# State products in four quarters, logits summed beside the turn of x, maxima joined on GpSimd, more of w1a loaded in the attention

## The chip, the cores and the metric

The kernel runs on one core of a Trainium2 chip. Its time is the device time of one execution in microseconds; the median of three runs stands for it. TensorE is called PE, VectorE DVE, ScalarE ACT, GpSimd POOL; SyncE (SP) issues nearly all loads.

## What is computed

Three layers follow one another, all in float32 at the outside.

```python
# 1. retention: 4 sequences, 8 heads, 768 tokens, 64 values a head
state = gamma[h] * state + outer(k[t], v[t])        # per head, 64 x 64
y[t] = q[t] @ state / sqrt(64)
x = y as (3072 tokens, 512)
# 2. soft mixture: 8 experts of 4 slots
logits = x @ phi                                    # 3072 x 32
d = softmax(logits, over the tokens); c = softmax(logits, over the slots)
slot_in = d.T @ x                                   # 32 x 512
slot_out[e] = relu(slot_in[e] @ w1[e]) @ w2[e]      # w1a, w2a in the kernel
x = c @ slot_out
# 3. top-2 mixture of 8 experts with noisy gates
out = sum of the two chosen experts' relu(x @ w1[e]) @ w2[e], weighted   # w1b, w2b
```

## The kernel before

**Tiling.** Tokens go in NT = 24 chunks of P = 128, six (NC) a sequence. Layer 1 works a chunk at a time: scores of keys against queries within the chunk, masked; the decayed v by the masked scores (`probs`), plus the state by the queries; then the state's update. Heads lie in pairs: partitions 0 to 63 hold the even head of pair n, 64 to 127 the odd one, so a state product contracts 64 rows into 64 columns.

**Order on TensorE.** It is written out by hand in `sequence_products` (L735). Step t does, in this order: `scores` of chunk t+1 (L643), `logit_parts_of` chunk t-1 (L657: phi by x, one part for each 128 values, in four column groups of 32), `turn_x` of t-1 (L675, four transposes, behind a wait for the state), at a few steps `turn_max` (L704) and `spread_max` (L710), `outputs` of t (L684 the state products, L690 v by probs), `logit_rows` of t-1 (L664, which adds the four parts by a stack of unit matrices), `update` of t (L697; not for a sequence's last chunk). In three steps `slot_sums` and `den_sums` (L719, L731) follow: sums over the tokens of exp(logits) by x, for one group of chunks. There are five groups (0 to 3, 4 to 7, 8 to 13, 14 to 19, 20 to 23), each with the running maximum of its columns; older sums are faded to the new maximum.

**Other engines in a step.** DVE: scales and decays the output into `x_t` (L1189), brings the state forward (L1198, L1201), masks the scores of t+2 (L1182). The column maximum of a group is four things: a reduce and a copy on DVE (L1222, L1224), a transpose on PE, a reduce, a join and a diagonal on DVE (L1230 to L1233), a product on PE that spreads it, then the shift (L1241). ACT copies the parts (L1009), the turned x (L1015) and the logits (L1017) out of the PSUM banks, and takes the exponentials. POOL decays v of t+2 once chunk t's v is used up (`decay_chunk`, L531), in a loop of the engine, and is free of other work until the attention ends. Its first partition all-reduce stands in `w2b_all_sum` (L564).

**Loads.** All go through one SP queue in the order of the program: for each chunk g the queries and keys half (`load_qk`) and the turned keys and v half (`load_kv`), 512 KB each, as soon as their buffers are free (four and two deep: the second waits for scores and the decay of v of chunk g-2), and behind them halves of w1a's units, 1 MB each, evenly spread: 14 over the chunks 3 to 23. A unit is 2 MB, 16 KB in each of 128 partitions; `w_region` holds eight, `s_region` two. The eighth unit of w1a has its home in unit 3, where the attention keeps its input chunks, so its second half is loaded when those two buffers are free and the first half after the last scores. Then come w2a's units (their homes are freed by the w1a products, `ring_used`), w1b's and w2b's.

**Behind the attention.** The w1a products (L808), the w2a products (L830), the softmax over the slots and the gates, the choice of two experts and sorting of tokens, mostly on DVE, the w1b weights folded with the slots (L866), and a loop over RT = 55 tiles (L940, L957) in which POOL fetches records and writes and adds rows by indirect transfers (L588, L594, L600).

## Time and profile before

| | us |
|---|---|
| timed, median of three runs (564.08 to 568.5) | 565.28 |
| span of the profiled execution | 563.3 |
| PE busy | 515.7 (92%) |
| DVE busy | 277.4 (49%) |
| POOL busy | 257.3 (46%) |
| ACT busy | 187.4 (33%) |
| moved by the DMA engines | 107.91 MB, mean 192 GB/s |

The profile is one execution. Its views show busy time in stretches, instructions in order of time with the idle time ahead of them and what ended it, and the chain of work that ended last. A product in float32 is two instructions in the profile. The DMA share is the mean busy share of 16 DMA engines. The attention runs from about 5 us to 134 us, the w1a and w2a products to 185 us, gates and sorting to 241 us, the tile loop to the end.

### The profile page before, as it was taken

The page shows a single profiled execution, that of the slowest core. Times are in us where ns is not written, and L with a number is a line of the kernel's source. Part 1 is how long each engine was busy: PE and PEld are TensorE (multiplying, and loading weights), DVE is VectorE, ACT ScalarE, POOL GpSimd, SP SyncE. Part 2 cuts the span into 40 slices and gives each one's busy share as a digit, 9 for nine tenths or more (in the row PEclk, how much of TensorE's full clock was granted, in tenths as well). Part 3 has the DMA queues.
Part 4 walks back from the last instruction along what each step waited for, and adds up shares of the span by engine and source line. Part 5 has one row for each costly group of instructions (what it writes and reads, how often), then busy time and mean ns, then how long its engine had stood idle before and what let it go on. Part 6 is the DMA issues. An engine that isn't in the chain of part 4 may idle for free.

```text
span 563.3 us, 13506 instructions
## 1 busy us (share of the span) xinstructions
PE 515.7 (92%) x4845; PEld 305.0 (54%) x4846; DVE 277.4 (49%) x449; ACT 187.4 (33%) x345; POOL 257.3 (46%) x216
## 2 busy tenths in 40 slices
PE   4999999998895767789999999999999999999992
PEld 4787878775465534345545454545454545454541
DVE  1665756573710388863363637373737242424240
ACT  0122222222000354763636464545452222222220
POOL 1212221220100003735587778777778757566632
PEclk9999999999799578979999999999999999999998
DMA  7899999877899999915435552222232342424310
GB/s 261 308 324 392 313 353 340 334 287 266 347 430 424 427 400 412 311 50 200 156 94 177 191 189 44 41 40 54 42 54 43 49 56 42 57 38 54 45 18 2
DMA packets 32358, 107.91 MB, mean 192 GB/s; under 512 B 11567, under 2 KB 12831, under 8 KB 27840
## 3 DMA queue, kind: packets, MB, share of 16 engines
q1 hardware_dynamic: 18144, 92.89, 43.5%
q0 software_dynamic: 14176, 14.49, 14.3%
q8 instruction: 26, 0.43, 0.3%
q14 instruction: 12, 0.10, 0.1%
HBM read 93.87 MB, written 29.43 MB: 219 GB/s over the span
## 4 chain that ended last, share of the span: by engine, by line
PE 82%; DVE 7%; DMA 4%; issue 3%; ACT 1%; POOL 1%; SPq 0%; DVEq 0%; POOLq 0%
PE ps L957 49%; PE ps L940 4%; PE ps L690 4%; PE ps L643 4%; PE ps L684 3%; PE ps L808 3%; PE ps L830 3%; PE ps L675 3%; PE ps L697 2%; DMA w_region<-chunks 2%; DMA w_region<-moe_w 2%; PE ps L664 1%; PE ps L657 1%; PE ps L719 1%; ACT r_region L1067 1%
## 5 line engine op out<-in xcount | busy, mean ns | idle before, releaser
L957 PE MATMUL ps<-w_region,s_region 128*128 (+1 forms) x1320 | 296.1, 381 | 1.1 <-ACT s_region L1136 1.1
L957 PEld LDWEIGHTS ps<-w_region,s_region 128*128 128x128 f16 x1320 | 127.4, 98 | 145.7 <-issue 4.2
L1559 DVE SCALAR_TENSOR_TENSOR s_region<-ps,s_region 128x1024 f16<-128x1024 f32 x55 | 67.3, 1224 | 148.4 <-ACT s_region L1136 148.3
L1136 ACT ACTIVATE s_region<-ps 128x1024 f16<-128x1024 f32 x55 | 56.3, 1023 | 183.2 <-PE ps L940 178.8
L594 POOL DMA_INDIRECT out<-s_region,rec_region x41 | 56.1, 1367 | 53.2 <-DVE s_region L1588 50.0
L600 POOL DMA_INDIRECT out<-s_region,rec_region x42 | 67.8, 1614 | 16.4 <-issue 12.0
L588 POOL DMA_INDIRECT rec_region<-records,idx x55 | 60.0, 1090 | 24.9 <-issue 16.3
L531 POOL TENSOR_TENSOR s_region<-w_region,s_region 128x512 f32<-128x512 f32 x22 | 22.9, 1042 | 90.5 <-PE ps L697 71.7
L940 PEld LDWEIGHTS ps<-s_region,sw_region 128*128 (+1 forms) x440 | 29.4, 98 | 15.3 <-issue 2.7
L1588 DVE TENSOR_SCALAR s_region<-ps,rec_region,y_scale 128x512 f32<-128x512 f32 x42 | 33.8, 804 | 6.9 <-PE ps L957 5.4
L940 PE MATMUL ps<-s_region,sw_region 128*128 128x128 f16 x440 | 34.1, 221 | 2.0 <-ACT sw_region L1089 2.0
L1189 DVE TENSOR_TENSOR sw_region<-ps,s_region 128x512 f32<-128x512 f32 x24 | 16.6, 692 | 35.0 <-PE ps L690 35.0
L1360 DVE SCALAR_TENSOR_TENSOR w_region<-w_region,w2b_scale 128x2048 f16<-128x2048 f32 x14 | 32.6, 2342 | 0.0
L564 POOL PARTITION_ALL_REDUCE w2b_sum<-w2b_sum x8 | 3.2, 402 | 56.6 <-ACT w_region L1067 55.9
L1049 ACT ACTIVATE w_region<-w_region,w2b_scale 128x2048 f16<-128x2048 f32 x14 | 27.8, 2001 | 0.7 <-DVE w2b_scale L1354 0.7
L594 POOL DMA_INDIRECT out<-r_region,rec_region x13 | 19.5, 1504 | 16.4 <-DVE r_region L1588 15.6
L1009 ACT ACTIVATE s_region<-ps 128x128 f32<-128x128 f32 x24 | 6.7, 277 | 52.8 <-PE ps L657 52.8
L1067 ACT ACTIVATE r_region<-w_region 128x2048 f16<-128x2048 f32 x12 | 22.9, 1912 | 0.5 <-DMA w_region<-moe_w 0.4
L600 POOL DMA_INDIRECT out<-r_region,rec_region x13 | 20.7, 1592 | 4.8 <-issue 3.7
L643 PE MATMUL ps<-w_region 64*128 64x128 f32 x192 | 15.8, 310 | 5.1 <-DMA w_region<-chunks 5.0
L1182 DVE TENSOR_TENSOR sw_region<-ps,s_region 128x512 f32<-128x512 f32 x24 | 15.4, 680 | 9.2 <-PE ps L643 9.2
L1182 DVE TENSOR_TENSOR s_region<-ps,s_region 128x512 f32<-128x512 f32 x24 | 15.4, 681 | 6.5 <-PE ps L643 6.5
(241 smaller groups left out, 576.4 us busy)
## 6 DMA issues: line engine op xcount, KB each, us to landing
w_region<-moe_w SPq DMA_DIRECT2D x11, 2048.0 KB, 10.0
w_region<-chunks SPq DMA_DIRECT2D x34, 512.0 KB, 6.5
w_region<-moe_w SPq DMA_DIRECT2D x16, 1024.0 KB, 9.2
w_region<-moe_w SPq DMA_DIRECT2D x24, 512.0 KB, 17.1
s_region<-moe_w SPq DMA_DIRECT2D x4, 2048.0 KB, 16.8
sw_region<-chunks SPq DMA_DIRECT2D x12, 512.0 KB, 6.2
s_region<-moe_w SPq DMA_DIRECT2D x2, 1024.0 KB, 8.0
s_region<-moe_w SPq DMA_DIRECT2D x1, 1536.0 KB, 6.5
```

The lines of the kernel that those rows point to most:

```text
L588: nc.gpsimd.indirect_dma_start(rec_i[:, i * RW:(i + 1) * RW], None, records[:, :], bass.IndirectOffsetOnAxis(ap=idx[:, i:i + 1], axis=0), ...
L594: nc.gpsimd.indirect_dma_start(out[:, :], bass.IndirectOffsetOnAxis(ap=rec_i[:, i * RW + SL + 1:i * RW + SL + 2], axis=0), y_sb[i % DEPTH] ...
L600: nc.gpsimd.indirect_dma_start(out[:, :], bass.IndirectOffsetOnAxis(ap=rec_i[:, i * RW + SL + 2:i * RW + SL + 3], axis=0), y_sb[i % DEPTH] ...
L643: last = nc.tensor.matmul(bank[SC[c % 2][i]][:, n * P:(n + 1) * P], kt_in[g % KV_DEPTH][rows, n, :], qt_in[g % QK_DEPTH][rows, n, :], star ...
L940: last = nc.tensor.matmul(bank[2 + 2 * r + f // 4][:, f % 4 * P:(f % 4 + 1) * P], sw_parts[:, bass.ds(e, 1), f * P:(f + 1) * P].rearrange( ...
L957: last = nc.tensor.matmul(bank[6 + r], h[:, r, f, :], w2b_parts[:, bass.ds(o, 1), part, f, :].rearrange("p e m -> p (e m)"), start=(first ...
L1067: nc.scalar.activation(unused, w2b_in[e][:, part * UNIT // W2B_SUMS:(part + 1) * UNIT // W2B_SUMS], ACT.Abs, accum_out=w2b_sum[:, 0, e, pa ...
L1136: nc.scalar.activation(h_hi[:, r, :, :].rearrange("p c t -> p (c t)").rearrange("p (a n) -> p a n", a=2), ps[:, 2 + 2 * r:4 + 2 * r, :], A ...
L1182: last = nc.vector.tensor_tensor(probs[c % 2][:, i, :, :], bank[SC[c % 2][i]][:, :].rearrange("p (n t) -> p n t", n=NP), causal[:, :].unsq ...
L1360: last = nc.vector.scalar_tensor_tensor(out=w2b_parts[:, e, 1, chunks, :], in0=w2b_in[e].rearrange("p (c m) -> p c m", c=FC)[:, chunks, :] ...
L1559: nc.vector.scalar_tensor_tensor(out=h_lo[:, r, :, :].rearrange("p c t -> p (c t)").rearrange("p (a n) -> p a n", a=2), in0=ps[:, 2 + 2 * ...
L1588: nc.vector.tensor_scalar(y_sb[r], bank[6 + u % 2], rec[:, bass.ds(i * RW + SL, 1)], y_scale[:, bass.ds(o, 1)], ALU.mult, ALU.mult).then_i ...
```

## The change

- **Quarters.** The output of the attention lies in two PSUM banks, Y and Y+1, 256 columns each, instead of one. The state product of head (row half i, pair n = 2m + half) goes to column half `half` of bank Y + i, so that four products in a row use four different 64x64 quarters of the array. The values of x come out in another order; the constants, phi and w1a's rows are laid out to match on the host.
- **Logits.** The parts lie beside the outputs in bank Y+1, the row sums beside the state in bank ST. The row sum of chunk t-2 follows the turn of x of chunk t-1 (before: that of t-1 followed the outputs of t), from one of two buffers. The wait for the state moves from ahead of the turn to behind it. New waits: the outputs wait for the copy of the parts, the update for the copy of the logits, ACT for the older row sum.
- **Maxima.** DVE's reduce is followed by one partition all-reduce on POOL (in the order of `decay_chunk`, behind chunks 6, 10, 16 and 22, whose loop is now unrolled, and once after the attention), DVE's maximum with the older one and the shift. The fade comes from the difference of two maxima, picked by three small DVE operations behind the shift. PE's transpose and spread go.
- **Loads.** A new region `late_w1a` of 12 KB a partition takes three quarters of w1a's eighth unit in two pieces (1 MB and 512 KB) spread with the others, 16 pieces over the chunks 3 to 23; the last quarter is loaded to unit 3 when its buffers are free. Behind the last scores, where w1a's half was loaded, three quarters of w2a's eighth unit are loaded to unit 3; only its last quarter waits for the w1a products.
- **Rings.** The space that POOL's transfers are described in (`dynamic_dma_scratch_size`) is set to 4 KB a partition, which makes room for the region.

The core of the diff; the rest follows from it (names of semaphores, buffers, and the waits ahead of the w1a and w2a products).

```diff
...
+        LATE = 3 * UNIT // 4
...
+        late_w1a = sb("late_w1a", [P, LATE], F32)
...
-        Y, ST, T_X, LG = range(4, 8)
+        Y, T_X, ST = 4, 6, 7
+        y_of = [bank[Y + i][:, 0:2 * P] for i in range(2)]
+        y_all = ps[:, Y:Y + 2, 0:2 * P]
+        parts_at = bank[Y + 1][:, 2 * P:3 * P]
+        den_at = bank[Y + 1][:, 400:402]
+        state_at = bank[ST][:, 0:NP * D]
+        rows_at = bank[ST][:, NP * D:NP * D + SL]
...
-                more = (g - 2) * 2 * (E - 1) // (NT - 3)
+                more = (g - 2) * 2 * E // (NT - 3)
                 for half in range(ahead, more):
-                    w1a_half(half // 2, half % 2, w1a_early)
+                    if half < 2 * (E - 1):
+                        w1a_half(half // 2, half % 2)
+                    elif half == 2 * (E - 1):
+                        late_w1a_words(0, HALF)
+                    else:
+                        late_w1a_words(HALF, LATE)
                 ahead = more
...
-            w1a_half(E - 1, 1, w1a_last_full)
+            sp.dma_start(w1a_home[E - 1][:, LATE:UNIT], w1a[E - 1, :, LATE:UNIT]).then_inc(w1a_last_full, 16)
             sp.wait_ge(scores_ready, NT)
             sp.wait_ge(v_decayed, NT)
-            w1a_half(E - 1, 0, w1a_last_full)
+            load_w2a_words(E - 1, 0, LATE)
...
-            for c in range(2, NC):
-                decay_chunk(0, c)
-            with pool.Fori(1, B) as b:
-                for c in range(NC):
-                    decay_chunk(b, c)
+            def join_col_max(g):
+                pool.wait_ge(col_max_ready, g + 1)
+                nc.gpsimd.partition_all_reduce(col_max[:, 1 if g > 0 else 2, :], col_max[:, 0, :], P, MAX).then_inc(col_max_joined, 1)
+
+            for t in range(2, NT):
+                decay_chunk(t // NC, t % NC)
+                for g in group_ending(t - 2):
+                    join_col_max(g)
...
             pool.wait_ge(x_turned, NT)
             nc.gpsimd.memset(in_blocks, 0.0).then_inc(blocks_zeroed, 1)
+            join_col_max(NG - 1)
...
-            def logit_rows(b, c):
-
-                pe.wait_ge(parts_kept, b * NC + c + 1)
-                nc.tensor.matmul(bank[LG][:, P:P + SL], logit_parts, stack, start=True, stop=True).then_inc(logits_done, 1)
...
+            def logit_rows(t):
+
+                pe.wait_ge(parts_kept, t + 1)
+                if t > 0:
+                    pe.wait_ge(logits_kept, t)
+                nc.tensor.matmul(rows_at, logit_parts[t % 2], stack, start=True, stop=True).then_inc(logits_done, 1)
...
             def outputs(b, c):
 
+                t = b * NC + c
+                if t > 0:
+
+                    pe.wait_ge(parts_kept, t)
                 if c > 0:
-                    for n in range(NP):
-                        for i in range(2):
-                            part = slice(i * D, (i + 1) * D)
-                            nc.tensor.matmul(bank[Y][part, n * P:(n + 1) * P], state[part, n, :],
-                                             qt_in[(b * NC + c) % QK_DEPTH][part, n, :],
-                                             start=(n == 0), stop=False, skip_group_check=True)
-                pe.wait_ge(v_decayed, b * NC + c + 1)
-                pe.wait_ge(probs_ready, b * NC + c + 1)
+                    for m in range(2):
+                        for half in range(2):
+                            for i in range(2):
+                                rows, n = slice(i * D, (i + 1) * D), 2 * m + half
+                                nc.tensor.matmul(y_of[i][half * D:(half + 1) * D, m * P:(m + 1) * P], state[rows, n, :],
+                                                 qt_in[t % QK_DEPTH][rows, n, :],
+                                                 start=(m == 0), stop=False, skip_group_check=True)
+                pe.wait_ge(v_decayed, t + 1)
+                pe.wait_ge(probs_ready, t + 1)
+                for m in range(2):
+                    for i in range(2):
+                        for half in range(2):
+                            n = 2 * m + half
+                            h = 2 * n + i
+                            last = nc.tensor.matmul(y_of[i][half * D:(half + 1) * D, m * P:(m + 1) * P],
+                                                    v_dec[c % 2][:, h * D:(h + 1) * D], probs[c % 2][:, i, n, :],
+                                                    start=(c == 0 and m == 0), stop=(m == 1), skip_group_check=True)
+                last.then_inc(y_ready, 1)
+
+            def update(b, c):
+                t = b * NC + c
+                if t > 1:
+
+                    pe.wait_ge(logits_kept, t - 1)
                 for h in range(H):
-                    last = nc.tensor.matmul(bank[Y][h % 2 * D:(h % 2 + 1) * D, h // 2 * P:(h // 2 + 1) * P],
-                                            v_dec[c % 2][:, h * D:(h + 1) * D], probs[c % 2][:, h % 2, h // 2, :],
-                                            start=(c == 0 and h < 2), stop=(h >= H - 2), skip_group_check=True)
-                last.then_inc(y_ready, 1)
-
-            def update(b, c):
-                for h in range(H):
-                    last = nc.tensor.matmul(bank[ST][h % 2 * D:(h % 2 + 1) * D, h // 2 * D:(h // 2 + 1) * D],
-                                            k_in[(b * NC + c) % QK_DEPTH][:, h * D:(h + 1) * D], v_dec[c % 2][:, h * D:(h + 1) * D],
+                    last = nc.tensor.matmul(state_at[h % 2 * D:(h % 2 + 1) * D, h // 2 * D:(h // 2 + 1) * D],
+                                            k_in[t % QK_DEPTH][:, h * D:(h + 1) * D], v_dec[c % 2][:, h * D:(h + 1) * D],
                                             start=(h < 2), stop=(h >= H - 2), skip_group_check=True)
                 last.then_inc(update_done, 1)
...
-                    if c > 0 or b > 0:
-                        logit_parts_of(before_b, before_c)
-                        if c > 0:
-
-                            pe.wait_ge(state_ready, b * (NC - 1) + c)
-                        turn_x(before_b, before_c)
-                    t = b * NC + c
-                    for g in group_ending(t - 1):
-                        turn_max(g)
-                    for g in group_ending(t - 2):
-                        spread_max(g)
+                    logit_parts_of(t - 1)
+                    turn_x(t - 1)
+                    if c > 0:
+
+                        pe.wait_ge(state_ready, b * (NC - 1) + c)
+                    if t > 1:
+                        logit_rows(t - 2)
                     outputs(b, c)
-                    if c > 0 or b > 0:
-                        logit_rows(before_b, before_c)
                     if c < NC - 1:
-                        for g in group_ending(t - 1) + (group_ending(t - 2) if c == 0 else []):
-
-                            pe.wait_ge(max_diag_ready, g + 1)
-                        for g in group_ending(t - 2) + (group_ending(t - 3) if c == 0 else []):
-
-                            pe.wait_ge(cols_shifted, g + 1)
                         update(b, c)
                     for g in group_ending(t - 3):
                         if g < NG - 2:
                             slot_sums(g, range(GROUPS[g][1] - GROUPS[g][0]), bank[T_X], t)
...
-            logit_parts_of(B - 1, NC - 1)
-            turn_x(B - 1, NC - 1)
-            logit_rows(B - 1, NC - 1)
-
-
-            slot_sums(NG - 2, range(REP), bank[0], GROUPS[NG - 2][1])
-            turn_max(NG - 1)
-            slot_sums(NG - 2, range(REP, GROUPS[NG - 2][1] - GROUPS[NG - 2][0]), bank[0], GROUPS[NG - 2][1])
+            logit_parts_of(NT - 1)
+            logit_rows(NT - 2)
+            turn_x(NT - 1)
+            logit_rows(NT - 1)
+
+
+            slot_sums(NG - 2, range(GROUPS[NG - 2][1] - GROUPS[NG - 2][0]), bank[0], GROUPS[NG - 2][1])
             den_sums(NG - 2, NT)
...
+            def keep_logits(t):
+                act.wait_ge(logits_done, t + 1)
+                nc.scalar.activation(logits[:, t, :], rows_at, ACT.Copy).then_inc(logits_kept, 1)
+
+            def keep_chunk(t):
+                act.wait_ge(parts_done, t + 1)
+                if t > 1:
+
+                    act.wait_ge(logits_done, t - 1)
+                nc.scalar.activation(logit_parts[t % 2], parts_at, ACT.Copy).then_inc(parts_kept, 1)
                 for n in range(NG - 2):
-                    if GROUPS[n][0] == g - len(x_ring):
+                    if GROUPS[n][0] == t - len(x_ring):
 
                         act.wait_ge(slot_in_done, n + 1)
-                act.wait_ge(x_turned, g + 1)
-                nc.scalar.activation(x_home(g), bank[T_X][:, :], ACT.Copy).then_inc(x_kept, 1)
-                act.wait_ge(logits_done, g + 1)
-                nc.scalar.activation(logits[:, g, :], bank[LG][:, P:P + SL], ACT.Copy).then_inc(logits_kept, 1)
+                if t == NT - 1:
+                    keep_logits(t - 1)
...
+                if 0 < t < NT - 1:
+                    keep_logits(t - 1)
...
+            def max_at(g):
+                return col_max[:, 2 + g % 2, :]
+
+            def shift_cols(g):
+                dve.wait_ge(col_max_joined, g + 1)
                 if g > 0:
+                    link(nc.vector.tensor_tensor(max_at(g), col_max[:, 1, :], max_at(g - 1), ALU.max))
                 if 0 < g < NG - 1:
 
                     dve.wait_ge(den_kept, g)
                 nc.vector.tensor_tensor(exp_of(g), logits[:, GROUPS[g][0]:GROUPS[g][1], :],
-                                        bank[ST][:, 3 * P:3 * P + SL].unsqueeze(1)
-                                        .to_broadcast([P, GROUPS[g][1] - GROUPS[g][0], SL]),
+                                        max_at(g).unsqueeze(1).to_broadcast([P, GROUPS[g][1] - GROUPS[g][0], SL]),
                                         ALU.subtract).then_inc(cols_shifted, 1)
+                if g > 0:
+                    dve.wait_ge(ident_full, 16)
+                    link(nc.vector.tensor_tensor(gap_stack, max_at(g - 1), max_at(g), ALU.subtract))
+                    link(nc.vector.tensor_tensor(gap_stack, gap_stack, stack, ALU.mult))
+                    nc.vector.tensor_reduce(gap[:, g:g + 1], gap_stack, AX_X, ALU.add).then_inc(gap_found, 1)
...
-                        join_max(g)
+                        find_max(g)
                     for g in group_ending(t - 2):
                         shift_cols(g)
                     keep_x_t(b, c)
-                    for g in group_ending(t):
-                        find_max(g)
...
-    y_decay = (power / np.sqrt(D)).reshape(H // 2, 2, 1, P).repeat(D, 2).reshape(H // 2, P, P).transpose(1, 0, 2)
+    y_decay = (power / np.sqrt(D)).reshape(H // 4, 2, 2, P).transpose(1, 2, 0, 3)[:, None].repeat(D, 1).reshape(P, H // 2, P)
...
-    nc = bacc.Bacc("TRN2", target_bir_lowering=False, num_devices=1)
+    nc = bacc.Bacc("TRN2", target_bir_lowering=False, num_devices=1, dynamic_dma_scratch_size=4096)
...
+    for name in ("moe_phi", "moe_w1"):
+        arrays[name] = by_quarter(arrays[name], inputs["q"].shape[1])
...
```

## Rows read from the trace of the kernel before

**Rows 1.** Windows: us, busy (instructions) by engine, PEclk, DMA share, GB/s.

```profile
20.00:120.00 100.00, 99.40 (x1495) 78.44 (x1491) 62.39 (x111) 22.08 (x66) 20.71 (x20) 1.00 0.95 348
20.00:30.00 10.00, 9.83 (x154) 7.81 (x152) 6.58 (x10) 2.14 (x6) 2.08 (x2) 1.00 1.00 387
150.00:182.50 32.50, 25.18 (x676) 19.19 (x669) 5.56 (x20) 0.87 (x2) 0.00 (x0) 1.00 1.01 426
```

**Rows 2.** The chain that ended last, tile loop: start us, us, what.

```profile
307.67 5.18 PE ps L957 x24
...
313.35 5.18 PE ps L957 x24
```

**Rows 3.** Timeline of step 3: start us, us, engine line op, shapes [idle before <-releaser].

```profile
26.57 1.16 PE L643 MATMUL ps<-w_region 64*128 64x128 f32 x16
...
27.15 0.97 DVE L1201 TENSOR_TENSOR s_region<-s_region 128x256 f32<-128x256 f32 x1
...
28.17 0.42 PEld L675 LDWEIGHTS ps<-ident_stack,sw_region 128*128 128x128 f32 x4 [0.35 <-DVE s_region L1201]
...
28.76 0.85 PEld L684 LDWEIGHTS ps<-sw_region,s_region 64*64 64x64 f32 x16 [0.17 <-issue]
...
29.78 1.09 PE L690 MATMUL ps<-s_region 128*64 128x128 f32 x16
...
30.81 0.41 PE L664 MATMUL ps<-ident_stack,s_region 128*128 128x32 f32 x2
...
31.14 0.69 PE L697 MATMUL ps<-s_region,sw_region 128*64 128x64 f32 x16
...
31.76 0.38 PE L643 MATMUL ps<-w_region 64*128 64x128 f32 x2
```

**Rows 4.** The chain that ended last, w2a products (L830).

```profile
161.78 5.45 PE ps L830 x192
...
170.06 3.70 PE ps L830 x128
...
182.47 2.36 PE ps L830 x36
```

**Rows 5.** The chain that ended last, end of the attention.

```profile
121.12 0.11 PE ps L704
...
124.23 1.09 PE ps L643 x16
...
126.36 0.33 PE ps L710 x2
...
133.42 0.70 DVE sw_region L1189
...
143.26 2.77 PE ps L808 x21
```

**Rows 6.** POOL's timeline, and the instructions of L543 and L564 (ns min/median/max).

```profile
10.15 0.28 POOL L543 TENSOR_SCALAR_AFFINE_SELECT before<-before 128x128 f32<-128x128 f32 x1 [8.71 <-issue]
...
37.11 1.04 POOL L531 TENSOR_TENSOR s_region<-w_region,s_region 128x512 f32<-128x512 f32 x1 [4.08 <-PE ps L697]
...
L543 POOLq MODIFY_POOL_CONFIG  x2: 11/11/11, 1.5 to 1.5; - x2
...
L564 POOL PARTITION_ALL_REDUCE w2b_sum<-w2b_sum x8: 312/323/872, 198.2 to 408.3; - x8
L564 POOLq MODIFY_POOL_CONFIG  x2: 11/14/16, 142.5 to 142.5; - x2
```

**Rows 7.** The page's DMA issues: count, size of one, median us to landing.

```profile
w_region<-chunks SPq DMA_DIRECT2D x34, 512.0 KB, 6.5
```

**Rows 8.** POOL's timeline in the tile loop.

```profile
302.46 1.59 POOL L600 DMA_INDIRECT out<-s_region,rec_region  x1 [1.79 <-DMA out<-s_region,rec_region]
304.35 1.05 POOL L588 DMA_INDIRECT rec_region<-records,idx  x1 [0.30 <-issue]
305.71 1.04 POOL L594 DMA_INDIRECT out<-s_region,rec_region  x1 [0.30 <-issue]
```

More of the change, by code:

```diff
@@ L98, in build_program @@
         ident_at = y_dec_at + NP * P
-        logit_parts = work_tile(3, P)
+        logit_parts = [work_tile(3, P) for _ in range(2)]
         x_ring = [w_region[:, 7 * UNIT + i * DM:7 * UNIT + (i + 1) * DM] for i in range(UNIT // DM)] + [work_tile(3, DM)]
@@ L436, in _, with w1a_half, late_w1a_words @@
             HALF = UNIT // 2
-            def w1a_half(e, half, full):
+            def w1a_half(e, half):
                 words = slice(half * HALF, (half + 1) * HALF)
-                sp.dma_start(w1a_home[e][:, words], w1a[e, :, words]).then_inc(full, 16)
+                sp.dma_start(w1a_home[e][:, words], w1a[e, :, words]).then_inc(w1a_early, 16)
+            def late_w1a_words(first, last):
+                sp.dma_start(late_w1a[:, first:last], w1a[E - 1, :, first:last]).then_inc(w1a_early, 16)
             ahead = 0
@@ L645, in scores, with logit_parts_of @@
                 last.then_inc(scores_ready, 1)
-            def logit_parts_of(b, c):
-                pe.wait_ge(x_t_ready, b * NC + c + 1)
-                if not (isinstance(b, int) and b * NC + c == 0):
-                    pe.wait_ge(logits_kept, b * NC + c)
-                for g in group_ending(b * NC + c - 3):
+            def logit_parts_of(t):
+                pe.wait_ge(x_t_ready, t + 1)
+                if t > 0:
+                    pe.wait_ge(parts_kept, t)
+                for g in group_ending(t - 3):
                     if g < NG - 2:
@@ L722, in slot_sums, with den_sums @@
                     last.then_inc(slot_in_done, 1)
-            def den_sums(g, kept):
-                pe.wait_ge(logits_kept, kept)
+            def den_sums(g, read):
+                pe.wait_ge(x_t_ready, read)
                 if g == NG - 1:
@@ L730, in den_sums @@
                 for c in range(end - first):
-                    last = nc.tensor.matmul(bank[LG][c % REP * SL:(c % REP + 1) * SL, 480:482], exp_of(g)[:, c, :],
+                    last = nc.tensor.matmul(den_at[c % REP * SL:(c % REP + 1) * SL, :], exp_of(g)[:, c, :],
                                             ones[:, 0:2], start=(c < REP), stop=(c >= end - first - REP))
@@ L825, in _ @@
                 for f in range(FC):
-                    if e == E - 1 and f == FC // 2:
+                    if e == E - 1 and (f + 1) * DM > LATE:
                         pe.wait_ge(w2a_last_full, 16)
```

101 lines of the change are left out of this document (42 added, 59 removed).

## The prediction

> **What bounds the kernel now.** I read the windows first, then the timeline of one step, then the chain. From 20 to 120 us TensorE is busy 99.40 of 100 us [rows 1]: the attention is a TensorE loop with no hole. The same row has the DMA engines at 0.95, moving 348 GB/s. So the first question is not what TensorE saves but what the loads allow. Behind the attention the order turns round: the DMA share is 1.01 at 426 GB/s from 150 to 182.5, with TensorE busy 25.18 of 32.50 us [rows 1]. The products with w2a wait for their weights there. In the last stretch, the loop over 55 tiles, TensorE takes one tile per 5.68 us (307.67 to 313.35) [rows 2], and the change does not touch it.
>
> **One step of the attention.** Starts in [rows 3]: scores and logit parts 1.61 us, turn of x 0.58, state products 1.02, v by probs 1.03, logit rows 0.33, update 0.62, together 5.19. Three prices are read off it. A change of the tile shape costs an idle 0.17 (ahead of L684). The turn waits 0.35 for the state on VectorE (L675), 0.18 more than such a switch. Sixteen 64x64 state products take 1.02 us, 64 ns each, two running side by side.
>
> **Part 1, state products in quarters.** The sixteen instructions stay; their order and banks make four neighbours use four different quarters (row half i, column half `half`, bank Y+i). The trace has no four 64x64 quarters at once. The nearest row is four column groups of 32: 128 products of 128 columns in 3.70 us, 28.9 ns each [rows 4]. Sixteen by 28.9 ns are 0.46 us; I take 0.49 with the last one's tail, a saving of 0.53. The other end is no overlap beyond today's two: saving 0. I take the upper one, because the nearest row has the same columns and type. VectorE reads 512 columns a chunk as before, now from two banks, at the same 0.69 us, and waits for nothing new.
>
> **Part 2, logits.** The row sum (L664) of the chunk before goes right behind the turn, which has its shape, so one 0.17 switch of the 0.33 disappears; I take 0.15. Its input was copied a step ago. New on TensorE's queue is the wait of the outputs for ScalarE's copy of the parts, which lies under the turn's 0.58; ScalarE is busy only 22.08 of 100 us [rows 1]. If that cover went, 0.1 to 0.3 a step. The wait for the state now stands behind the turn instead of ahead of it, so the 0.17 or so goes too: VectorE finished at 28.12, the turn ends at 28.76 [rows 3]. With steps 0.85 shorter it still fits, since parts and turn follow the scores.
>
> An ordinary step is then 5.19 - 0.53 - 0.15 - 0.17 = 4.34 us of TensorE. Up to the last scores at 124.23 [rows 5] there are 18 steps with state products (9.5 us), 20 row sums (3.0), about 15 waits for the state (2.6). Part 3 adds 1.4. Sum 16.5: **by TensorE alone the last scores would start at 107.7.**
>
> **Part 3, maxima on POOL.** Three spreads of 0.33 (the fourth is in the tail) and four turns of 0.11 leave TensorE's queue [rows 5]: 1.4 us. VectorE loses copies and the join and gains three small operations behind the shift, under 0.8 us in front of x in four steps, which its idle time takes (62.39 of 100 us busy [rows 1]). Added on POOL is a partition all-reduce, 0.3 to 0.9 us, and something that comes ahead of the first one. The trace has two events that reconfigure POOL: at 1.5, after which its next instruction starts at 10.15 behind 8.71 us of idle time, and at 142.5, ahead of the first all-reduce, where a 56 us wait hid it [rows 6]. In the changed kernel the second comes in the middle of the attention. Queued behind it are the decay of v for chunk 7 (which frees the load of chunk 9) and, by the join, VectorE's shift and its x of chunk 6. Worked out: decay 6 ends at 38.15 today [rows 6], about 35.6 once four steps have saved their part, plus 8.7 is 44.3, all-reduce, shift and x end at 45.8; TensorE would want that x at 43.6. A stall of 2.2 us, once. Loads already queued cover some; I count 1.6. The bounds are 0 (if the load takes under 6.5 us) and 2.2.
> The Trainium skill, GPSIMD Engine Reference, 2.1 Instruction dispatch, says that the first call of a freshly loaded kernel pays about 6 us (5.95 measured) of code load with no visible instruction. By it the stall would be nil and the sum 1.6 us better; the row here has 8.71, and the row decides.
>
> **Part 4, three quarters of w1a's eighth unit early.** Ahead of the last chunk the SP queue now carries 15 pieces of w1a instead of 13, 2.1 MB more. So from 20 us on, 34.8 + 2.1 = 36.9 MB must land before the last scores. What rate? The whole 100 us gave 348 GB/s at 0.95, or 366 at a full share. But the ten microseconds with the engines full (20 to 30) gave 387, and 150 to 182.5 gave 426 [rows 1]. A half-megabyte load takes 6.5 us from issue to landing [rows 7], far more than its bytes need, so a share counted busy with few loads queued need not mean a full pipe. With loads always queued I take 395, nearer to the 387, since the mix is the same; 366 and 426 are the ends. 36.9 MB / 395 GB/s = 93.4 us: landed at 113.4, with 1.0 for the hand-over 114.4, with POOL's 1.6 **116.0**. That is later than TensorE's 107.7, so the loads decide, and the gain at the last scores is 124.2 - 116.0 = 8.2 us rather than 16.5.
> The tail from there to the last x is 9.9 us now (124.23 to 134.12) [rows 5]; two state products (1.06), one spread (0.33) and two row switches (0.3) leave it: 1.7. **The attention ends 9.9 us earlier.**
>
> **Behind the attention.** 1.57 MB of w1a no longer need moving there: in their place and time w2a's eighth unit loads, whose three quarters the stretch at 1.01 is then spared. 1.57 MB / 426 GB/s = 3.7 us. The path of the last maxima loses a turn and a spread (0.11 and 0.33) and two small operations of VectorE, about 1.2 us in all, but it ends at TensorE's w1a products, and what ends last is the w2a load, so I count 0. Check that TensorE doesn't become the bound: its w1a products would start 11 us before 143.26 [rows 5], its w2a products 11 us before 161.78, and the latter (eight times 64 at 28.9 ns, 14.8 us, and 0.8 for turns between) could end at 166.4, 18 us before 184.8; the loads allow 13.6 [rows 4]. What follows (gates, choice, records, second weights, 54 more tiles) shifts whole.
>
> **Rings of 4 KB.** By its name the space holds what POOL's own transfers need. Per tile POOL has 1.59 + 1.05 + 1.04 us and three gaps of 0.30, 4.6 of 5.68 us [rows 2, 8]. Room: 1.1 us a tile. I count 0; the cover is that room.
>
> **Sum.** 9.9 + 3.7 = 13.6. The profiled execution's span is 563.3, 2.0 below the median of the runs, 565.28; 549.7 of span, 551.7 timed.
>
> **Rivals.**
> *The loads hold at 366 GB/s.* For it: it is the rate of the whole stretch. Against: 387 and 426 in full windows. 36.9/366 = 100.8, so landed at 121.8, last scores at 124.4 or, with no stall, 122.8; gain 0 to 1.4, tail 1.7, w2a 3.7: about 559.
> The Trainium skill, DMA: Bandwidth & Descriptors, Where 436 GB/s comes from, says that HBM to SBUF is held to about 358 GB/s a core by HBM. That would be this rival, slightly worse; the trace's 426 over 32 us speaks against it for a single running core.
> *TensorE is the bound.* With 426 GB/s the loads land at 106.6, under TensorE's 107.7; with the stall 109.9, a gain of 14.3, then 1.7 and 3.7: 545.6. For it: the 426 of [rows 1], reached where loads are always queued. Against: over half of the bytes are chunk loads, which wait for buffers.
> *The quarters don't overlap.* TensorE alone: 124.2 - 7.0 = 117.2, with the stall 118.8; gain 5.4, tail 0.6, w2a 3.7: 555.6. It would be the change not doing what it says.
> *The attention gets no shorter*, because w1a's larger share ahead of the chunks in one queue delays them step by step: only 3.7 and perhaps 1: 561.
> *Slower: the small rings stall POOL.* If an indirect transfer has to wait for an earlier one's landing, and it costs POOL over 1.1 us a tile, each further microsecond is 54 us: with 1.79 (L600 waited that long for a DMA once already [rows 8]) 0.7 x 54 = 38, some 590. It decides from 1.1 us a tile; taken with the gain, from 1.35. Nothing else shows how full the rings are. A half clock in the attention would be slower too, but TensorE keeps a granted clock of 1.00, the 2.4 GHz level, in the window with 25.18 of 32.50 busy [rows 1], and the changed attention would leave it over 90% busy.
>
> **How the numbers follow.** Forecast (547 to 555) 0.45; quarters don't overlap 0.07; loads at 366 0.17; TensorE bound 0.12; attention no shorter 0.07; rings 0.07; slower otherwise 0.05. Leaving out the rings, the other slow cases and the lower end of the TensorE case, the range is 545 to 561. A per cent, 5.65 us, is about what a measurement of this kernel can tell. Faster than 559.6: 0.45 + 0.07 + 0.12 + half of the 366 case, 0.72. Within: the other half and the 561 case, 0.16. Slower 0.12.
>
> **What would show it.** In the profile after: L684's group at about 30 ns per instruction; an ordinary step of TensorE near 4.4 us of work inside a step of 4.6, with idle ahead of the scores put down to the chunk loads; a share of 0.99 or more and 385 to 405 GB/s from 20 to 110; one hole of 1 to 3 us near 44, with POOL idle some 8 us ahead of its first all-reduce; the last scores near 116; the w2a products' end at 171 instead of 184.8; POOL's rows in the tile loop unchanged. It is wrong if the scores don't wait for loads (then TensorE case), if the rate at full share stays below 375, or if tiles take over 5.68 us.

## The result and the profile after

| | before | after |
|---|---|---|
| median of the runs (lowest to highest), us | 564.68 (561.9 to 568.5, 4 runs) | 593.63 (591.25 to 596.68, 4 runs) |
| ratio to before, 95% interval | 1 | 1.051 [1.046, 1.057] |
| span of the profiled execution, us | 563.3 | 595.0 |
| mean granted clock of TensorE | 0.96 | 0.935 |

The change makes the kernel 5% slower: 593.6 us, where 551.7 was forecast. An execution over 1.5% above the fastest of its kernel is in a slower state of the chip and is left out of the medians below. The windows of the kernel after (us, busy us and instructions of PE, PEld, DVE, ACT and POOL, granted clock, DMA share, GB/s) answer to [rows 1]; the three short ones are holes, found with the next view:

```profile
20.00:120.00 100.00, 73.63 (x1186) 60.44 (x1182) 44.11 (x82) 15.61 (x50) 15.90 (x17) 0.90 0.77 291
...
50.00:57.00 7.00, 3.56 (x68) 2.88 (x64) 2.34 (x5) 1.27 (x4) 0.47 (x1) 0.96 0.02 7
...
78.00:87.00 9.00, 2.80 (x46) 2.11 (x46) 3.51 (x10) 1.48 (x5) 1.35 (x3) 0.82 0.05 17
...
120.00:127.00 7.00, 3.03 (x30) 2.19 (x30) 3.33 (x9) 1.53 (x5) 0.55 (x1) 0.59 0.00 0
```

TensorE, busy 99.40 of 100 us before, is busy 73.63, and the DMA engines move 291 GB/s instead of 348. In the holes next to nothing arrives. POOL's timeline says what they are (start, duration, engine, line, operation, idle time before it and what ended it):

```profile
49.25 0.45 POOL L572 PARTITION_ALL_REDUCE r_region<-r_region  x1 [11.31 <-issue]
56.53 2.04 POOL L545 TENSOR_TENSOR s_region<-w_region,s_region 128x512 f32<-128x512 f32 x2 [6.83 <-issue]
...
77.83 0.45 POOL L572 PARTITION_ALL_REDUCE r_region<-r_region  x1 [8.24 <-issue]
85.93 2.04 POOL L545 TENSOR_TENSOR s_region<-w_region,s_region 128x512 f32<-128x512 f32 x2 [7.65 <-issue]
...
119.23 0.45 POOL L572 PARTITION_ALL_REDUCE r_region<-r_region  x1 [10.26 <-issue]
126.45 2.04 POOL L545 TENSOR_TENSOR s_region<-w_region,s_region 128x512 f32<-128x512 f32 x2 [6.76 <-issue]
...
153.73 0.45 POOL L572 PARTITION_ALL_REDUCE r_region<-r_region  x1 [6.13 <-issue]
161.03 1.03 POOL L545 TENSOR_TENSOR s_region<-w_region,s_region 128x512 f32<-128x512 f32 x1 [6.84 <-issue]
...
174.80 0.45 POOL L572 PARTITION_ALL_REDUCE r_region<-r_region  x1 [6.88 <-issue]
```

The all-reduce itself takes 0.45 us. Ahead of every one of the five POOL stands idle for 6.1 to 11.3 us with no releaser, and ahead of the first multiplication of v behind four of them for 6.8 to 7.7 us more. The two lines' instructions show that POOL is reconfigured each time (count: ns min/median/max, first and last start):

```profile
L572 POOLq MODIFY_POOL_CONFIG  x10: 8/11/13, 38.1 to 168.1; - x10
...
L545 POOLq MODIFY_POOL_CONFIG  x8: 99/99/99, 49.7 to 154.2; - x8
```

Before, the same entries came twice in pairs, at 1.5 and 142.5 us [rows 6]; now these two lines alone have nine pairs. The gaps sum to 42.8 us ahead of the five all-reduces and 28.1 us ahead of the four multiplications. The chain of waits shows what hangs on one of them (start, length, what):

```profile
72.39 0.49 PE ps L730 x16
...
72.92 4.91 issue
77.83 0.15 POOL r_region L572
...
78.37 7.56 issue
85.93 1.04 POOL s_region L545
...
87.03 4.65 DMA w_region<-chunks
...
91.72 0.37 PE ps L661
```

TensorE goes on for a few products and stops. The multiplication of v also frees a chunk's buffer, so SP's queue stands too: from 20 to 170 us its `load_kv` waited for POOL 14 times, 64.3 us in all. When POOL is back, a load of 4.65 us has to land before TensorE starts again. One alternation costs two gaps and a refill.

Between the holes the kernel does what the change wanted. Starts of steps that wait for nothing, with the state products, in TensorE's part of the timeline (it answers to [rows 3]):

```profile
107.70 1.16 PE L661 MATMUL ps<-w_region 64*128 64x128 f32 x16
108.80 0.43 PE L675 MATMUL ps<-sw_region,s_region 128*32 128x128 f32 x8
109.15 0.66 PE L695 MATMUL ps<-ident_stack,sw_region 128*128 128x128 f32 x4
109.64 0.31 PE L684 MATMUL ps<-ident_stack,s_region 128*128 128x32 f32 x2
109.88 0.67 PE L709 MATMUL ps<-sw_region,s_region 64*64 64x128 f32 x16
110.48 1.09 PE L719 MATMUL ps<-s_region 128*64 128x128 f32 x16
111.40 0.64 PE L730 MATMUL ps<-s_region,sw_region 128*64 128x64 f32 x16
111.97 0.71 PE L661 MATMUL ps<-w_region 64*128 64x128 f32 x8
```

A step is 4.27 us (107.70 to 111.97) instead of 5.19, and the state products take 0.60 (109.88 to 110.48) instead of 1.02. But x of the last chunk ends at 164.7 us instead of 134.12 [rows 5], the w1a products start at 181.2 instead of 143.26, and the tile loop runs 35.3 us later (its third L952 group starts at 285.50, before at 250.18) at the old 5.68 us a tile [rows 2] (L952 and L969 are the former L940 and L957).

### The profile page after: what moved, and what is told of

Read it like the earlier page. It is cut to its first block, busy times and chain, and to the rows that moved or that the text cites. A ratio compares the mean times of both kernels' runs of the same rounds, so it can differ in the third digit from the quotient of the medians.

```text
span 595.0 us, 13497 instructions
## 1 busy us (share of the span) xinstructions
PE 507.7 (85%) x4830; PEld 301.2 (51%) x4831; DVE 271.9 (46%) x446; ACT 185.4 (31%) x345; POOL 259.0 (44%) x221
## 4 chain that ended last, share of the span: by engine, by line
PE 70%; issue 11%; DMA 9%; DVE 5%; POOL 3%; ACT 1%; SPq 0%; POOLq 0%; DVEq 0%
PE ps L969 47%; DMA w_region<-chunks 9%; PE ps L952 4%; PE ps L661 3%; PE ps L820 3%; PE ps L719 3%; PE ps L842 3%; PE ps L695 1%; POOL rec_region L606 1%; PE ps L709 1%; PE ps L730 1%; POOL s_region L545 1%; PE ps L675 1%; PE ps L903 1%; PE ps L741 1%
## 5 line engine op out<-in xcount | busy, mean ns | idle before, releaser
L969 PE MATMUL ps<-w_region,s_region 128*128 (+1 forms) x1320 | 295.3, 380 | 1.1 <-ACT s_region L1159 1.1
L969 PEld LDWEIGHTS ps<-w_region,s_region 128*128 128x128 f16 x1320 | 127.2, 98 | 145.1 <-issue 3.2
L612 POOL DMA_INDIRECT out<-s_region,rec_region x41 | 55.9, 1364 | 53.4 <-DVE s_region L1603 51.2
L618 POOL DMA_INDIRECT out<-s_region,rec_region x42 | 67.9, 1616 | 15.3 <-issue 12.2
L606 POOL DMA_INDIRECT rec_region<-records,idx x55 | 60.0, 1091 | 25.3 <-issue 16.3
L952 PEld LDWEIGHTS ps<-s_region,sw_region 128*128 (+1 forms) x440 | 29.4, 98 | 15.4 <-issue 2.7
L952 PE MATMUL ps<-s_region,sw_region 128*128 128x128 f16 x440 | 34.1, 220 | 2.0 <-ACT sw_region L1112 2.0
L719 PE MATMUL ps<-s_region 128*64 128x128 f32 x192 | 16.5, 326 | 16.2 <-POOL s_region L545 16.2
L661 PE MATMUL ps<-sw_region,w_region 64*128 64x128 f32 x192 | 15.8, 310 | 13.9 <-DMA w_region<-chunks 13.9
L612 POOL DMA_INDIRECT out<-r_region,rec_region x13 | 19.1, 1470 | 17.4 <-DVE r_region L1603 16.6
## 6 DMA issues: line engine op xcount, KB each, us to landing
s_region<-moe_w SPq DMA_DIRECT2D x2, 1024.0 KB, 10.1
```

What stands on the lines that cost most here:

```text
L606: nc.gpsimd.indirect_dma_start(rec_i[:, i * RW:(i + 1) * RW], None, records[:, :], bass.IndirectOffsetOnAxis(ap=idx[:, i:i + 1], axis=0), ...
L612: nc.gpsimd.indirect_dma_start(out[:, :], bass.IndirectOffsetOnAxis(ap=rec_i[:, i * RW + SL + 1:i * RW + SL + 2], axis=0), y_sb[i % DEPTH] ...
L618: nc.gpsimd.indirect_dma_start(out[:, :], bass.IndirectOffsetOnAxis(ap=rec_i[:, i * RW + SL + 2:i * RW + SL + 3], axis=0), y_sb[i % DEPTH] ...
L661: last = nc.tensor.matmul(bank[SC[c % 2][i]][:, n * P:(n + 1) * P], kt_in[g % KV_DEPTH][rows, n, :], qt_in[g % QK_DEPTH][rows, n, :], star ...
L719: last = nc.tensor.matmul(y_of[i][half * D:(half + 1) * D, m * P:(m + 1) * P], v_dec[c % 2][:, h * D:(h + 1) * D], probs[c % 2][:, i, n, : ...
L952: last = nc.tensor.matmul(bank[2 + 2 * r + f // 4][:, f % 4 * P:(f % 4 + 1) * P], sw_parts[:, bass.ds(e, 1), f * P:(f + 1) * P].rearrange( ...
```

## The experiments

**Is it the alternation?** The theory: POOL loads code at each change between the all-reduce and the multiplication of v, and that is the whole loss. The rivals: the quarters, the order on TensorE, the moved loads or the rings. Two kernels keep everything of the change but end the alternation, each from the other side. The first moves the multiplications to DVE (`decay_later` is the same `tensor_tensor` on that engine):

```diff
-            for t in range(2, NT):
-                decay_chunk(t // NC, t % NC)
-                for g in group_ending(t - 2):
-                    join_col_max(g)
+            for g in range(NG - 1):
+                join_col_max(g)
...
+                    if t + 2 < NT:
+                        decay_later(t + 2)
```

> The kernel after, but every multiplication of v by its decay runs on DVE (about 0.3 us each, placed ahead of the mask of a later chunk); POOL has nothing but the all-reduces between its setup and the end of the attention, so it loads the code of the all-reduce once. Theory (the nine loads of POOL's code are the loss): attention without the stalls of 6 to 11 us, total near 553 us, 548 to 560. Rival (the all-reduce itself, or the new order on TensorE, or the loads moved into the attention are the loss): no more than a few us off 594.

Measured 546.5 (543.19 to 547.43; the profiled execution took 551.69), ratio 0.967 [0.961, 0.973], just under the range expected. A multiplication of v takes 0.68 us on DVE, not 0.3. The second gives the maxima back to TensorE, with `turn_max`, `spread_max` and `join_max` as before, in columns 256 to 416 of bank Y:

> The kernel after, but the maxima go through TensorE again, as before (a turn of the column maxima, then a product that spreads them), in the columns that the new layout leaves free; POOL does only the multiplications of v and never changes its code in the attention. Quarters, logits beside the turn of x, rings of 4 KB and the three quarters of w1a's eighth unit stay. Theory (changes of POOL's code are the loss): near 553 us, 548 to 560, so that it agrees with the version that moves the multiplications instead. Rival (quarters, layout or the moved loads are the loss): stays above 575.

Measured 553.62 (551.95 to 558.15), ratio 0.982 [0.974, 0.989]. The fourth corner has neither on POOL:

> The fourth of the square: the maxima through TensorE and the multiplications of v on DVE, all else of the kernel after. The other three: both on POOL 594, maxima alone on POOL 547, multiplications alone on POOL 554. Theory (each move is worth something by itself and only the pair on POOL costs, about 44 us): 547 to 554. Rival (the multiplication on POOL was itself the cause, by its port or its latency, and the all-reduce is free): 547 as with the maxima on POOL, or below.

Measured 552.68 (551.67 to 558.89), ratio 0.976 [0.973, 0.980]. The square: both on POOL 593.6, maxima alone 546.5, multiplications alone 553.6, neither 552.7. If each were worth something by itself and no more, both would give 546.5 + 553.6 - 552.7 = 547.4. The pair costs the 46.2 us between that and 593.6 (44.7 if the four ratios to before are used), and only the pair. The quarters, the order on TensorE, the moved loads and the rings are in all four, so none of them is the loss. In the first version POOL's rows read:

```profile
40.52 0.46 POOL L572 PARTITION_ALL_REDUCE r_region<-r_region  x1 [28.56 <-DVE r_region L1246]
...
130.88 0.98 POOL L583 MEMSET sw_region<- 128x1056 f32 x1 [10.70 <-PE ps L693]
132.05 0.43 POOL L572 PARTITION_ALL_REDUCE r_region<-r_region  x1 [0.19 <-DVE r_region L1246]
```

Its one reconfigure pair for the all-reduce comes at 12.2 us, under POOL's idle time of 28.56 us. A memset between two all-reduces costs nothing: the next starts after 0.19 us.

**The price in the kernel before.** One all-reduce with an unused result is put into the multiplications of v, then two together, then three apart. The loop over chunks is written out for it, as in the kernel after and in the version with the maxima on TensorE, which has no loss:

```diff
-            for c in range(2, NC):
-                decay_chunk(0, c)
-            with pool.Fori(1, B) as b:
-                for c in range(NC):
-                    decay_chunk(b, c)
+            for t in range(2, NT):
+                decay_chunk(t // NC, t % NC)
+                if t in (12,):             # three apart: (6, 12, 18)
+                    nc.gpsimd.partition_all_reduce(spare_max[:, 1, :], ones[:, 0:SL], P, ABSMAX)
```

> The kernel before with one extra all-reduce over partitions on POOL (128x32, result unused) behind the multiplication of chunk 12, so in mid-attention, and the loop over chunks written out. Theory: it costs one load of the all-reduce's code and one load back to the multiplication's, 6 to 9 us each as in the trace after, less what v's chunks in hand cover: 8 to 16 us slower than before, 573 to 581. Rival (an all-reduce costs its own 0.45 us, or one load only): 0 to 6 us slower.

> The kernel before with two extra all-reduces on POOL back to back behind the multiplication of chunk 12 (results unused). One extra all-reduce there made the kernel 12.8 us slower. Theory (a load is paid at each change between the two codes, not for a call): 0 to 1 us more than with one, 576 to 579. Rival (every call of the all-reduce pays): about 7 to 13 us more than with one, 584 to 590.

> The kernel before with three extra all-reduces, behind the multiplications of chunks 6, 12 and 18. Theory (every return to the other code pays again): three times 12.8 us, 598 to 606. Rival (code once loaded stays at hand, so the first pair of loads is the dear one): 577 to 585.

Measured: one 576.51, ratio 1.022 [1.016, 1.028], 12.8 us over the 563.75 of the kernel before beside it; two together 576.0, ratio 1.020 [1.016, 1.024], 11.5 over 564.55; three apart 594.81, ratio 1.053 [1.049, 1.057], 30.3 over 564.55, so 10.1 each. A second call beside the first is free; every return is paid again. POOL with two together, then with three apart:

```profile
76.84 0.45 POOL L560 PARTITION_ALL_REDUCE spare_max<-ones  x1 [9.10 <-PE ps L698]
77.20 0.53 POOL L561 PARTITION_ALL_REDUCE spare_max<-ones  x1
85.36 2.04 POOL L532 TENSOR_TENSOR s_region<-w_region,s_region 128x512 f32<-128x512 f32 x2 [7.62 <-issue]
```

```profile
131.13 0.45 POOL L560 PARTITION_ALL_REDUCE spare_max<-ones  x1 [8.79 <-PE ps L697]
138.55 2.04 POOL L532 TENSOR_TENSOR s_region<-w_region,s_region 128x512 f32<-128x512 f32 x2 [6.96 <-issue]
```

The 9.10 and 8.79 are put down to TensorE, but these calls have no wait in the program, and the first one's reconfigure pair stands at 67.9 us, right behind the multiplication that ended at 67.74. I expected 598 to 606 for three and got less: 10.1 for a return. The 12.8 of the single one isn't clearly more, since its interval goes from 9 to 16 us. The kernel after has four returns, 10.0 us each if the 40.0 us between it and the version with the maxima on TensorE are shared out, the fifth load at its end among them.

**Does the code wait behind other loads?**

```diff
-                for half in range(ahead, more):
+                for half in range(0, 2 * E if g == NT - 1 else 0):
```

> The kernel after, but with all of w1a loaded behind the last chunk; the total is of no use. Read POOL's idle time for no reason of the trace ahead of the all-reduces (8.6 us on average in the kernel after) and ahead of the multiplications (7.0 us). Theory A (a load of code has a price of its own): the same within 1 us. Theory B (the code comes through the same DMA engines and waits behind w1a's loads): clearly shorter, 5 us or less each.

Neither was right as it stands. Six of the nine gaps lie in the stretch without w1a's loads. Ahead of the all-reduces they are 7.78, 7.17 and 7.82 us, with the chunks' loads running (DMA share 0.65), ahead of the multiplications 7.45, 6.83 and 7.65, with the DMA engines idle: mean 7.5. The three that fell under w1a's late loads are longer:

```profile
142.72 0.45 POOL L572 PARTITION_ALL_REDUCE r_region<-r_region  x1 [10.93 <-issue]
153.95 1.03 POOL L545 TENSOR_TENSOR s_region<-w_region,s_region 128x512 f32<-128x512 f32 x1 [10.78 <-issue]
170.76 0.45 POOL L572 PARTITION_ALL_REDUCE r_region<-r_region  x1 [9.79 <-issue]
```

The windows of the same kernel, for the stretch of the second:

```profile
143.00:154.00 11.00, 3.03 (x30) 2.18 (x30) 2.38 (x8) 1.53 (x5) 0.22 (x2) 0.50 1.01 421
```

That looks like 3 us more for full DMA engines. The kernel after speaks against a rule of that kind: its gap of 8.24 us lies in this window of it,

```profile
69.00:78.00 9.00, 8.27 (x156) 7.00 (x154) 4.39 (x8) 1.93 (x6) 0.76 (x2) 1.00 0.99 402
```

its last, of 6.88, has a share of 1.00 as well, and its longest, of 11.31, has 0.85. What all the traces share is this: the twelve gaps in which the DMA engines did nothing (share 0.04 or less) took 6.8 to 7.7 us, and those with loads running 6.1 to 11.3. So loads beside it sometimes come with a longer gap and sometimes not; what decides it stays open. The total, 593.79, is no measure, since 15 MB come late.

**TensorE alone.** The same edit in the version with the multiplications on DVE takes the loads' part out of the attention:

> The version with the multiplications of v on DVE, but all of w1a is loaded behind the last chunk of the attention; nothing else is changed, and the total is of no use, since 15 MB come late. Read the step and the start of the last scores. Theory (without w1a's loads TensorE alone sets the pace): ordinary steps of 4.3 us from the start, last scores at 107 to 109. Rival (something else than the loads holds the steps, a buffer or DVE): the last scores start at 115 or later as with the loads.

TensorE's timeline (it answers to the 124.23 of [rows 5]):

```profile
103.16 1.16 PE L659 MATMUL ps<-sw_region,w_region 64*128 64x128 f32 x16
...
107.42 1.16 PE L659 MATMUL ps<-sw_region,w_region 64*128 64x128 f32 x16
```

The last scores start at 107.42, a step is 4.26 (the total, 568.19, is no measure here either). With w1a's loads in their place, and nothing else different, they start at 121.31 behind waits for chunks. The loads hold the attention, not TensorE.

**Part 4 undone**, in the version with the multiplications on DVE (w1a's eighth unit behind the attention, as in the kernel before):

> The version with the multiplications of v on DVE, without part 4: w1a's eighth unit is loaded behind the attention again, in two halves, as in the kernel before. Theory (the loads hold the attention, and the same bytes move whichever side they are on): the last scores start about 4 us earlier than its 121.3, the products with w1a wait for the eighth unit instead, and the total is within 3 us of 547. Rival (three quarters more in the attention fill time in which the DMA engines had nothing to do, the 3.7 us of my sum for the stretch of w2a): 3 to 5 us slower, 550 to 552.

Measured 545.18 (544.54 to 547.42), ratio 0.962 [0.959, 0.966]: the last scores start 8.8 us earlier, at 112.51 (5.0 of it may be chance: another version with the same loads as the one at 121.31 had them at 116.30), and the total is not told apart from 546.5, within the 3 us that the theory allowed. Part of what the attention gives is taken back behind it. In the two profiled executions (547.42 and 551.69 us) the w2a products end at 167.9 and 175.6, and the third tile group starts at 235.78 and 240.04. The chain of waits of the version without part 4 leaves TensorE's w2a products at 161.5 and goes on over loads of weights:

```profile
163.74 27.14 DMA w_region<-moe_w
...
198.20 15.71 DMA w_region<-moe_w
```

**The order of the state products.** Two other orders, in the same version. The first puts the column halves outermost, as below; the second takes for `crossed` and `m` in two loops `half = (i + crossed) % 2`:

```diff
-                    for m in range(2):
-                        for half in range(2):
+                    for half in range(2):
+                        for m in range(2):
                             for i in range(2):
```

> The version with the multiplications of v on DVE, but of the state products consecutive ones share a half of TensorE's columns, so that at most two run side by side and not four. Theory (quarters give the shorter product and the loads hold the attention): the group of 16 takes 1.02 us and not 0.60; the total grows by 0 to 4 us, 547 to 551, since the steps wait for loads in places anyway. Rival (the order within the quarters has no part in it): 0.60 us still, and the same time.

> The version with the multiplications of v on DVE, and the state products in the order of the kernel before: each pair takes diagonal quarters of TensorE's array (row half 0 with column half 0, row half 1 with column half 1), here first the one diagonal and then the other, but each row half still writes a PSUM bank of its own. The order by halves of the columns left the group at 0.60 us. Theory (what the change gained lies in the bank of its own for each row half, not in the order of the quarters): 0.60 us again. Rival (diagonal pairs are the slow order): 1.02 us as in the kernel before.

The first took 547.62 (545.88 to 549.08), ratio 0.967 [0.962, 0.972]; the second, a single run, 549.52. The group ahead of the products with v, in the first and the second:

```profile
104.00 0.68 PE L707 MATMUL ps<-sw_region,s_region 64*64 64x128 f32 x16
104.61 0.85 PEld L717 LDWEIGHTS ps<-s_region 128*64 128x64 f32 x16 [0.17 <-issue]
```

```profile
106.97 0.68 PE L708 MATMUL ps<-sw_region,s_region 64*64 64x128 f32 x16
107.58 1.09 PE L718 MATMUL ps<-s_region 128*64 128x128 f32 x16
```

It is 0.61 us from start to start in both, and not the 1.02 that I expected of the first: four neighbours in four quarters aren't needed, and diagonal pairs like those of before aren't slow. What before has and none of these three orders has is both row halves writing one PSUM bank. The Trainium skill, TensorEngine Tiling (Array Packing), Gotcha 1: PSUM Pressure, says that row tiles have to write different banks to run at once; 1.02 us with one bank and 0.60 with two agree. That the bank is the cause is inferred by leaving the order out: the same order with one bank was not tried, because the two row halves would then write the same partitions of it unordered.

**The rings alone**, in the kernel before:

```diff
-num_devices=1)
+num_devices=1, dynamic_dma_scratch_size=4096)
```

> The kernel before with rings of 4 KB for descriptors and nothing else. Theory (the ring has no part in the loss): within 1% of before, 565 us. Rival (POOL's indirect DMAs of the tile loop wait for room in a small ring): 28 us slower than before and more, 590 to 600.

Measured 561.37, ratio 0.994 [0.992, 0.997]: no loss but a small gain. The chain's last row, of the kernel before and of this one:

```profile
core 0 of [0], span 563.3 us
...
554.50 1.57 POOL out L600
```

```profile
core 0 of [0], span 558.2 us
...
553.02 1.58 POOL out L600
```

From the end of POOL's last instruction to the end of the span it is 7.2 us before and 3.6 with the small rings. The tile loop keeps its 5.68 us a tile. The kernel after has this gain too (3.6 us).

## Why the prediction was wrong

**The step that failed is "A stall of 2.2 us, once".** I had the right event, a price near it (8.71 us; the first gap took 11.31, from the end of the multiplication for chunk 6 at 37.94 instead of 35.6) and the work queued behind it, and asked only when the all-reduce's code would come for the first time. The multiplication of chunk 7 that I named as queued behind it is the other kind of instruction: it needs the former code back, and the next all-reduce needs its own again. By the places of the five all-reduces that is nine loads, and the nearest price was at hand: four returns of twice 8.71 less what the buffers cover. The runs showed nine gaps, 70.9 us in sum, and 40.0 us of time over the version with the maxima on TensorE, against the 1.6 us that I counted. It belonged among the rivals with the decisive point "if POOL keeps one code at a time". My slower rival sat on POOL as well, but at the rings, which cost nothing. The Trainium skill, GPSIMD Engine Reference, 2.1 Instruction dispatch, speaks of the first call of a freshly loaded kernel; "freshly loaded" happens here at every change, at 6.1 to 11.3 us against its 5.95.

**TensorE's part came out right in the sum.** Forecast were steps of 4.34 us and last scores at 107.7 by TensorE alone; measured 4.27, and 107.42 without w1a's loads. That it fits so well is partly luck: the state products saved 0.42 instead of 0.53, the rest of the step 0.50 instead of 0.32, 0.11 of it in v by probs, for which I had counted nothing. That neighbours in four quarters are what does it was wrong, the banks suffice as far as tried.

**The rate of the loads was sized too high.** 395 GB/s was taken, with 366 as a rival. The version with the maxima on TensorE shows it, from 20 to 120 us:

```profile
20.00:120.00 100.00, 88.51 (x1509) 73.12 (x1509) 61.89 (x111) 20.46 (x67) 20.84 (x20) 0.98 0.98 369
```

It is 369 GB/s at a share of 0.98. The five versions with the multiplications on DVE and w1a's loads in the attention have 361 to 381 at 0.96 to 0.99. None reaches 395, and they spread by 20 among themselves, nearly as much as the 29 between my figure and the rival's. This version's last scores start at 122.90 and not at 116.0. The rival had 122.8 without a stall, but its sum counts the hand-over of 1.0 twice: 20 + 100.8 + 1.0 is 121.8. With a share of 0.98 the DMA engines had next to no idle time left, so I was wrong to expect more GB/s from loads that are always queued.

**Behind the attention.** That version's w2a products end at 179.2 instead of 184.8, a gain of 5.6. Its tile loop starts 6.2 us earlier (third L974 group at 243.96), its closing is 3.6 shorter: 9.9 of span, and 553.6 against the forecast 551.7. That this is close is partly luck: the loads gave 7 us less, the closing 3.6 that I did not have in the sum. Part 4 as such, counted at 3.7, is worth nothing that can be measured, with the multiplications on DVE: without it the kernel is at 545.2, with it at 546.5. The bytes that have to arrive are the same.

**What the parts are worth.** The rings 2 to 3 us. Parts 1 and 2 with part 4, from the rings' 561.4 to 553.6 or 552.7: 8 to 9, from a step shorter by 0.9 of which the loads take back most. In the profiled executions the last scores start at 122.89 with the rings alone and at 122.90 with the other parts too; the whole 4.8 us between these two spans arise behind them. The maxima on POOL, with the multiplications away from it, from 552.7 to 546.5: about 6, four times what I gave to the spreads and turns (1.4). VectorE's part of the join and the waits of TensorE for it go as well, but that they make up the difference isn't shown. The two best versions, the multiplications on DVE with part 4 (546.5) and without (545.2), beat both kernels; they are not told apart.

## What to carry to other kernels

Before an operation goes to POOL, list what POOL does around it in program order and count the changes between kinds of code, not the first use: a change took 6 to 11 us here, so keep one kind in a loop, or put the changes where POOL idles anyway. Read POOL's reconfigure entries in the trace; here each load had one pair of them. And in a stretch with the DMA share at 0.95 and above, price a faster engine at what the bytes allow at the measured rate of that mix of transfers (361 to 381 GB/s here), not at the best rate of another.

## What the runs showed of the hardware

- In this kernel POOL was reconfigured at every change between the all-reduce and the multiplication, in both directions: 6.1 to 11.3 us each, 6.8 to 7.7 in the twelve cases with idle DMA engines. A second all-reduce behind the first had no gap, and one behind a memset 0.19 us.
- A change and back, with the refill of the chunk buffers behind it, cost 10.0 to 12.8 us of the kernel's time.
- TensorE's granted clock fell where POOL let it stand idle. It did nothing from 40.70 to 44.96 us; from 44 to 48 us the clock was 0.50, the 1.2 GHz level, and the scores at 44.96 took 2.08 us instead of 1.16. From 120 to 127 us it was 0.59.
- Rings of 4 KB for descriptors made the closing 3.6 us shorter, and no transfer of the tile loop slower (L612 1364 ns, L618 1616, L606 1091; before 1367, 1614, 1090). Why the closing gets shorter is open.
- Sixteen 64x64 products took 0.60 or 0.61 us in three orders with a PSUM bank for each row half, and 1.02 with both in one.
